# Nine groups of 256 tokens in place of six of 384 in a fused attention and two-MLP kernel

## What is computed

```python
def _attn_ref(q, k, v):                      # (4, 8, 576, 64), in chunks of 64 tokens
    scores = scale * np.matmul(q_c, k_c.transpose(0, 1, 2, 4, 3))
    scores = scores - np.max(scores, axis=-1, keepdims=True)
    attn = np.exp(scores)
    attn = attn / (np.sum(attn, axis=-1, keepdims=True) + 1e-09)
    return np.matmul(attn, v_c)
def _moe_ref(x, w_in, w_out):                # (2304, 512), (512, 2048), (2048, 512)
    h = x @ w_in
    return (h - np.tanh(h)) @ w_out
def _moe2_ref(x, w_in, w_out):
    h = x @ w_in
    sp = np.where(h > 20.0, h, np.log1p(np.exp(np.minimum(h, 20.0))))
    return (h * np.tanh(sp)) @ w_out
# out = _moe2_ref(_moe_ref(attention, first weights), second weights)
```

## Time and profile before

| what | value |
|---|---|
| times of two runs | 859.07 and 860.32 us, median 859.7 |
| span of the profiled execution, from its first to its last instruction | 859.9 us |
| TensorE matmul, busy | 844.7 us, 98% |
| VectorE, busy | 477.4 us, 56% |
| ScalarE, busy | 384.9 us, 45% |
| GpSimd, busy | 42.1 us, 5% |
| moved by DMA | 36.1 MB, mean 42 GB/s |
| matmuls | 5544 |

### The profile page before, as it was taken

How to read it: one execution, slowest core, us unless ns; L and a number is a source line. 1 busy time by engine, 2 the same in 40 slices (tenths; PEclk the granted TensorE clock), 3 DMA queues, 4 the chain that set the end, 5 groups by cost and what they waited for, 6 DMA issues and landing times.

```text
span 859.9 us, 14387 instructions
## 1 busy us (share of the span) xinstructions
PE 844.7 (98%) x5544; PEld 794.8 (92%) x5544; DVE 477.4 (56%) x878; ACT 384.9 (45%) x736; POOL 42.1 (5%) x70
## 2 busy tenths in 40 slices
PE   4999999999999999999999999999999999999998
PEld 3999999999999999999999999999999999999997
DVE  5656533443353343344558667667667667667664
ACT  4544332333243233333446555445446545445553
POOL 3230000000000000011331000000000000000000
PEclk9999999999999999999999999999999999999999
DMA  7452111011101100111341001000000000000100
GB/s 247 168 161 64 37 37 31 21 37 37 37 24 37 37 26 23 37 49 35 123 138 50 1 0 37 1 1 37 0 0 36 1 0 0 37 0 1 38 1 37
DMA packets 15360, 36.10 MB, mean 42 GB/s; under 512 B 2016, under 2 KB 2016, under 8 KB 15328
## 3 DMA queue, kind: packets, MB, share of 16 engines
q1 hardware_dynamic: 10208, 18.88, 6.7%
q0 software_dynamic: 5120, 16.78, 5.9%
HBM read 30.93 MB, written 4.72 MB: 41 GB/s over the span
## 4 chain that ended last, share of the span: by engine, by line
PE 97%; DMA 1%; DVE 0%; ACT 0%; SPq 0%; issue 0%; DVEq 0%
PE psum L608 15%; PE psum L610 15%; PE psum L609 15%; PE psum L637 8%; PE psum L638 8%; PE psum L623 8%; PE psum L622 8%; PE psum L621 8%; PE psum L636 8%; PE psum L554 1%; PE psum L583 1%; PE psum L598 1%; PE psum L599 1%; PE psum L603 1%; PE psum L566 1%; DMA y_all<-kT 1%
## 5 line engine op out<-in xcount | busy, mean ns | idle before, releaser
L608 PE MATMUL psum<-x_hi,w_hi 128*128 128x384 f32 x720 | 246.3, 342 | 0.0
L610 PE MATMUL psum<-x_hi,w_lo 128*128 128x384 f32 x720 | 241.7, 336 | 0.0
L609 PE MATMUL psum<-x_lo,w_hi 128*128 128x384 f32 x720 | 241.3, 335 | 0.0
L430 DVE TENSOR_TENSOR act_a<-psum,act_a 128x384 f32<-128x384 f32 x96 | 53.4, 557 | 166.4 <-ACT act_a L272 166.4
L608 PEld LDWEIGHTS psum<-x_hi,w_hi 128*128 128x128 f32 x720 | 135.4, 188 | 5.9
L609 PEld LDWEIGHTS psum<-x_lo,w_hi 128*128 128x128 f32 x720 | 135.4, 188 | 3.8
L610 PEld LDWEIGHTS psum<-x_hi,w_lo 128*128 128x128 f32 x720 | 135.1, 188 | 0.0
L623 PE MATMUL psum<-g_hi,w_lo 128*128 128x384 f32 x384 | 128.4, 334 | 0.0
L621 PE MATMUL psum<-g_hi,w_hi 128*128 128x384 f32 x384 | 128.3, 334 | 0.0
L622 PE MATMUL psum<-g_lo,w_hi 128*128 128x384 f32 x384 | 128.3, 334 | 0.0
L483 DVE TENSOR_SCALAR act_a<-psum 128x384 f32<-128x384 f32 x96 | 53.5, 557 | 116.1 <-PE psum L610 116.1
(11 more groups left out here) (65 smaller groups left out, 893.8 us busy)
## 6 DMA issues: line engine op xcount, KB each, us to landing
region<-v SPq DMA_DIRECT2D x17, 256.0 KB, 2.7
region<-qT SPq DMA_DIRECT2D x16, 256.0 KB, 2.7
region<-kT SPq DMA_DIRECT2D x16, 256.0 KB, 2.9
y_all<-w POOLq DMA_DIRECT2D x16, 256.0 KB, 3.6
y_all<-w_out POOLq DMA_DIRECT2D x16, 256.0 KB, 4.0
region<-w POOLq DMA_DIRECT2D x16, 256.0 KB, 3.3
region<-w_out POOLq DMA_DIRECT2D x16, 256.0 KB, 3.2
out<-region SPq DMA_DIRECT2D x5, 768.0 KB, 3.5
```

The costliest lines, as they stand in the source:

```text
L430: dve.tensor_tensor(act_a[:, f % 2, :], h_ps[f % 2][:, 0:GROUP], act_a[:, f % 2, :], ALU.subtract).then_inc(g_done, 1)
L608: pe.matmul(ps, w_hi[:, f, 0, cols], x_hi[:, k, :], start=k == 0, stop=False)
L609: pe.matmul(ps, w_hi[:, f, 0, cols], x_lo[:, k, :], start=False, stop=False)
L610: mm = pe.matmul(ps, w_lo[:, f, 0, cols], x_hi[:, k, :], start=False, stop=k == KT - 1)
```

## The change

A group becomes two tiles, 256 tokens, and there are nine groups. The operations on a group's tokens keep their form with 256 columns in place of 384; `y2` has two output tiles in place of three, so 6 matmuls a step. Two tiles of attention are done ahead of the MLP, and two in each first-MLP group but the last, six steps apart, with turn three steps behind scores and values two behind turn. What belonged to the third tile ahead of the MLP (its semaphore, its buffers, its places in the streams) is gone. Outputs are written in eight DMAs of two tiles and two of one.

```diff
-GROUP_TILES = 3
+GROUP_TILES = 2
-SCORES_AT = {1 + 5 * i: i for i in range(GROUP_TILES)}
-TURN_AT = {3 + 5 * i: i for i in range(GROUP_TILES)}
-VALUES_AT = {4 + 5 * i: i for i in range(GROUP_TILES)}
+SCORES_AT = {1 + 6 * i: i for i in range(GROUP_TILES)}
+TURN_AT = {4 + 6 * i: i for i in range(GROUP_TILES)}
+VALUES_AT = {6 + 6 * i: i for i in range(GROUP_TILES)}
...
-        views_2 = qk_views(spare[:, 5 * words:]) + views[2:]
...
-            return {1: views_1, 2: views_2}.get(t, views) if isinstance(t, int) else views
+            return views_1 if isinstance(t, int) and t == 1 else views
...
-            first = 2 * t - 2 if isinstance(t, int) and t in (1, 2) else 6
+            first = 0 if isinstance(t, int) and t == 1 else 6
...
             load_qk(1, qk_loaded_1)
-            load_qk(2, qk_loaded_2)
             load_v(0)
             load_v(1, v_loaded_1)
-            sp.wait_ge(values_ready, 1)
-            load_v(2)
...
             exps(1)
             copy_turned(0)
-            exps(2)
             split_chunk_hi(1)
             keep_x(0, 0, 0)
             copy_turned(1)
-            copy_turned(2)
             split_chunk_hi(2)
             keep_x(1, 1, 0)
-            keep_x(2, 2, 0)
...
-                for j in range(2):
-                    act.activation(out_sb[:, j, :], y_ps[j][:, :], ACT.Copy).then_inc(outputs_read, 1)
+                act.activation(out_sb[:, 0, :], y_ps[0][:, :], ACT.Copy).then_inc(outputs_read, 1)
...
             shift(1)
-            shift(2)
             normalise(1)
-            normalise(2)
...
-                dve.tensor_copy(out_sb[:, 2, :], y_ps[2][:, :]).then_inc(outputs_read, 1)
+                dve.tensor_copy(out_sb[:, 1, :], y_ps[1][:, :]).then_inc(outputs_read, 1)
...
             turn(1)
-            turn(2)
             wait_for_values(1)
             values(1)
-            wait_for_values(2)
-            values(2)
             hidden(0, 0, 2, None)
```

More of the change, by code:

```diff
@@ L110, in build @@
         spare = y_words[:, STAGE1 * 2 * D_MODEL:]
-        assert 7 * words <= spare.shape[1] and 5 * words <= region.shape[1]
+        assert 5 * words <= spare.shape[1] and 5 * words <= region.shape[1]
         views = qk_views(region) + rest_views(region[:, 2 * words:])
         views_1 = qk_views(spare) + rest_views(spare[:, 2 * words:])
-        views_2 = qk_views(spare[:, 5 * words:]) + views[2:]
         def views_of(t):
-            return {1: views_1, 2: views_2}.get(t, views) if isinstance(t, int) else views
+            return views_1 if isinstance(t, int) and t == 1 else views
         stage2 = region[:, 0:STAGE2 * 2 * D_MODEL].rearrange("p (r n) -> p r n", r=STAGE2)
@@ L135, in attention_banks @@
         def attention_banks(t):
-            first = 2 * t - 2 if isinstance(t, int) and t in (1, 2) else 6
+            first = 0 if isinstance(t, int) and t == 1 else 6
             return psum[:, first:first + 2, 0:256], psum[:, first:first + 2, 256:512]
         qk_loaded, v_loaded = sem("qk_loaded"), sem("v_loaded")
-        qk_loaded_1, v_loaded_1, qk_loaded_2 = sem("qk_loaded_1"), sem("v_loaded_1"), sem("qk_loaded_2")
+        qk_loaded_1, v_loaded_1 = sem("qk_loaded_1"), sem("v_loaded_1")
         stage1_loaded = [sem(f"stage1_loaded{i}") for i in range(STAGE1)]
@@ L249, in copy_turned @@
                 if not (isinstance(t, int) and t < 2):
-                    act.wait_ge(values_ready, 1 if isinstance(t, int) and t == 2 else t)
+                    act.wait_ge(values_ready, t)
                 act.activation(views_of(t)[4], attention_banks(t)[1], ACT.Copy).then_inc(turned_copied, 1)
@@ L381, in _ @@
             act.wait_ge(out_sb_free, 16 * GROUPS)
-            for j in (0, 2):
-                act.wait_ge(last_ready, j + 1)
-                act.activation(out_sb[:, j, :], y_ps[j][:, :], ACT.Copy).then_inc(last_read[j], 1)
+            act.wait_ge(last_ready, 1)
+            act.activation(out_sb[:, 0, :], y_ps[0][:, :], ACT.Copy).then_inc(last_read[0], 1)
         @block.vector
@@ L404, in shift @@
                 if not (isinstance(t, int) and t < 2):
-                    dve.wait_ge(turned, (t - 1) if isinstance(t, int) and t == 2 else t)
+                    dve.wait_ge(turned, t)
                 dve.tensor_tensor(probs, scores, row_max[:, :, :].unsqueeze(3).broadcast_to((P, 2, 4, CHUNK)),
@@ L541, in wait_for_scores @@
             def wait_for_scores(t):
-                if isinstance(t, int) and t in (1, 2):
-                    pe.wait_ge(qk_loaded_1 if t == 1 else qk_loaded_2, 32)
+                if isinstance(t, int) and t == 1:
+                    pe.wait_ge(qk_loaded_1, 32)
                 else:
-                    pe.wait_ge(qk_loaded, 32 if isinstance(t, int) and t == 0 else 32 * (t - 1))
+                    pe.wait_ge(qk_loaded, 32 if isinstance(t, int) and t == 0 else 32 * t)
                 if not (isinstance(t, int) and t < GROUP_TILES):
```

## The result

The changed kernel takes 891.8 us, median of two runs (890.83 and 892.76), against 859.7: the ratio is 1.037, with a 95% interval of 1.0335 to 1.0405. The forecast was 892.2, in a range of 879 to 908. One of the five executions of a later kernel (y2 in halves) took 2945 us, for a reason that nothing on record shows, and is left out of its ratio.

A forecast was written before the change was run, and what follows sets the result against it. TensorE's matmul stream, busy 98% of 859.9 us, was taken as the bound. Adding 23.0, 1.6, 2.1, -3.1, 3.2, 5, 0.5 and 0.2 gave 892.4, and 892.2 us as forecast time, range 879 to 908.

The forecast's parts named there:

- 1728 more matmuls: TensorE, hidden and y1: more matmuls for the same streamed columns, each paying 13.3 ns beside its columns, +23.0 us.
- second-MLP surplus: TensorE in the second MLP: slightly longer matmul distances, 1.07 us a group before the change, would add +1.6 us.
- one tile more in the stream: Attention on TensorE: the third tile moves into the stream, 16 in place of 15 at 2.11 us, +2.1 us.
- shorter start: Before the MLP: with two tiles ahead, TensorE begins hidden near 18.5 in place of 21.65, -3.1 us (-2 to -4.2).
- first group: First first-MLP group: TensorE waits for VectorE's low weight splits, 2.2 us and then 1.0, +3.2 us (1 to 6).
- weight ring, entry to the second MLP: Last first-MLP group: two-place weight ring takes 6.8 us for two chunks against two steps of 5.76, +5 us (2 to 10).
- where second-MLP groups meet, end: VectorE's last x_lo is late, eight times 0.06 to 0.1 us, +0.5; y2's last input is late, +0.2.
- rival (a): TensorE: matmul distance goes with the columns, 0.1156 us at 256, so the 23 us fall away: 869.3; chance 0.07.
- The load's floor: TensorE: a 128x128 weight load, 0.11 us apart in the rows, fits under the 120 ns of a 256-column matmul.
- rival (d): Waits are larger than walked: the ring's landing grows or TensorE's clock falls in the waits; 900 to 908, chance 0.13.
- (b): TensorE: a small fixed part under 4.5 ns a matmul, at most 7.8 us for the 23: 869 to 877; chance 0.03.
- (e): The waits don't arise, as the lag of two steps between hidden and y1 takes them all: 884; chance 0.12.

The follow-up runs named there:

- y2 in halves: Kernel before the change, with y2's 512-column matmuls issued as two of 256, but for the first and last of each sum: 864.8 us, ratio 1.0045.
- the ladder: Kernel before the change, with 24 extra matmuls of each of nine shapes behind its last y2: 226.7 ns at 512 columns, 119.8 at 256, 110.9 at 192.
- three places: Changed kernel with three places in place of two in the staging ring of the second MLP's weights: 886.2 us, ratio 1.0302.
- the other order: Changed kernel with the first group's weight split, in steps with attention, ahead of exps on ScalarE and shift on VectorE: 888.6 us, ratio 1.0329.
- the run with both changes: Changed kernel with three places in the second MLP's weight ring and the first group's weight splits ahead of exps and shift: 882.1 us, ratio 1.0254.
- y1 in halves: Kernel before the change, with y1's 384-column matmuls issued as two of 192, but for the first and last of each sum: 928.3 us.

## Why the prediction was right

The median came out 0.4 us off, which is closer than the terms are. The prediction's sum, 892.4, was one of spans, and against the span of 891.0 it is 1.4 off; it took span and time for the same, where the time is 1.8 higher. By terms, from the profiled executions (859.9 and 891.0):

| term | forecast | measured | from |
|---|---|---|---|
| 1728 more matmuls | +23.0 | +23.0 | 0.120 us a distance in the first MLP; the ladder |
| second-MLP surplus | +1.6 | -3.5 | 45.33 - 192 x 0.120 - 96 x 0.2267 = 0.53, of it 0.21 for x_lo; 0.32 x 9 against 1.07 x 6 |
| one tile more in the stream | +2.1 | +1.3 | (50.20 - 46.08) / 2 = 2.06 a tile, x 16, less 15 x 2.11 |
| shorter start | -3.1 | -4.05 | 17.60 against 21.65 |
| first group | +3.2 | +3.2 waits, +1.5 clock | 2.2 and 0.8, and 0.1 for the matmul behind each; 16 x 0.0933 |
| weight ring, entry to the second MLP | +5 | +5.4 waits, +1.5 clock | 5.0, and 0.4 for the matmuls behind; three places take 6.8 away |
| where second-MLP groups meet, end | +0.7 | +2.2 | 8 x 0.21, and 0.5 at the end |

The measured column gives 859.9 + 30.6 = 890.5, 0.5 short of the span.

*The matmuls.* The step that carried the forecast was reading two shapes where nothing else disturbs them and splitting the distance into columns and a rest. It measured 13.3 ns in the ladder and in the changed kernel. Between 512-column matmuls it is another price, as the run with y2 in halves shows, but the change splits none of those. Judged by the ratio of 384 to 256 columns alone, rival (a), or by the mixed stretches of the second MLP, it would have been missed. The load's floor was read as 0.11 us and is 0.112 in a settled stream, so 256 columns clear it by 8 ns. Narrower groups would gain nothing more: a 192-column matmul takes 112 ns.

*The waits.* The walk of the two queues gave the right places, producers and sizes: 2.2 us at VectorE's low split of chunk 4, 1.0 (0.79) at the next tile, and a ring of 6.8 us (6.76). The run with three places and the one with the other order took each away alone.

*Where it was off.* The clock, rival (d), did fall twice, 1.5 us each; the forecast had it outside the sum, and its 2 us for 4 us of half clock are a little too much, as a matmul at half clock takes 213.3 ns, without the 13.3. The waits where second-MLP groups meet were found in the right place but sized at 0.06 to 0.1 us, where each costs 0.21, half of it as a longer matmul behind the wait. The surplus had the wrong sign: I let it go with the steps or with the columns. A 512-column matmul pays 4.5 ns of it in both kernels; the other part was on the 384-column matmuls between them, 192 x 2.15 ns a group, and the 256-column matmuls that took their place don't pay it: leaving out the wait on x_lo, they are at 119.4. Why wide matmuls among narrower ones pay at all stays open. The third tile costs 0.05 less per tile in the stream. The start gained 0.9 more, inside the bounds given, as tile 1's shift began at 9.40 in place of 10.33. Part of that is chance: in the five other runs whose start is that of the kernel before, TensorE begins hidden between 20.6 and 22.2, and in the three others with the changed start between 17.35 and 18.0. The clock, the waits where groups meet and the longer matmuls behind waits (about +4.9) and surplus, tile and start (-6.9) go against each other, and the nearness of 892.2 to 891.8 owes that to luck.

*The other rivals.* (b) is excluded by the ladder. (e), no waits, is nearly what the run with both changes makes by hand: 21.1 us over the kernel before, where (e) had 24; surplus, tile and start account for the rest.

## What to carry to other kernels

On an engine that is full all the time, the price of smaller groups is the number of instructions times what each costs beside its data. Find that rest from two sizes of the same instruction in a quiet stretch, and find the floor from the shortest one. In a mixed stretch the price can be another, so measure it there as well. Then look for chores whose length doesn't shrink with the group (weight splits, ring loads): what two steps covered before, two shorter steps may not, and a ring of two is the first to show.

## What the runs showed of the hardware

- A matmul of these rounded operands with 128x128 weights took columns / 2.4 + 13.3 ns from 512 down to 256 columns, and 112 ns in a settled stream at 192, 128 and 64. With 64-column weights 128 and 256 columns took 59.9 and 113.3 ns, columns / 2.4 + 6.7. At half clock 256 and 384 columns took 213.3 and 320 ns, columns / 1.2 and nothing beside.
- 512-column matmuls among 384- or 256-column ones took 231.2 ns on average in place of 226.7, and the 384-column ones 175.5 in place of 173.3; in the ladder the first 384-column distances behind 512-column ones were 171, 175, 177, 185, 176 and 181 ns, with the other engines almost idle, before they settled at 173 to 174.
- Loops of 590 and 682 matmuls ran without instruction fetches in the trace; one of 774 fetched in every turn, in blocks of 16 KB, and stood twice at each turn, for 1.2 to 2.0 us.
- The first 256-column matmul behind a wait took 0.22 us in place of 0.120, in ten and more places.
- TensorE's clock fell to half for 3.41 us behind a distance of 2.34 us between two starts, and again behind one of 2.56; in the run with y1 in halves it fell behind one of 2.01, for 6.83 us, with a distance of 1.24 in them. It stayed full behind one of 1.80 (the run with the other order) and behind four of 1.77 to 1.89 (y1 in halves, later turns).
